# Four weight pieces' low parts formed by GpSimd instead of VectorE, beside the first batch's MLP

## What is computed

```python
def _moe2_ref(x, w_ch1, w_ch2) -> np.ndarray:
    X = np.fft.fft(x, axis=1)
    X = np.fft.fft(X, axis=2)
    mixed = np.real(X).astype(np.float32)
    u = x + mixed
    mu = np.mean(u, axis=-1, keepdims=True)
    var = np.mean((u - mu) ** 2, axis=-1, keepdims=True)
    un = (u - mu) / np.sqrt(var + 1e-06)
    ch = np.maximum(un @ w_ch1, 0.0) @ w_ch2
    return (u + ch).astype(np.float32)
```

## Time and profile before

| | us |
|---|---|
| median of 3 runs | 588.84 |
| lowest, highest | 588.84, 588.99 |
| the profiled execution, whole | 591.47 |
| its span, first to last instruction | 589.7 |

### The profile page before, as it was taken

One profiled execution on the slowest core, in us unless ns is written; L12 is line 12 of the kernel. 1 busy time (PEld: TensorE's weight loads), 2 busy tenths in 40 slices (PEclk: granted clock), 3 DMA queues, 4 the chain that ended last, 5 costly groups with the idle time before them and its releaser, 6 DMA issues.

```text
span 589.7 us, 12408 instructions
## 1 busy us (share of the span) xinstructions
PE 573.9 (97%) x5173; PEld 544.0 (92%) x5173; DVE 399.8 (68%) x891; ACT 199.1 (34%) x441; POOL 14.0 (2%) x31
## 2 busy tenths in 40 slices
PE   7999999999999999999999999999999999999996
PEld 6788999999999999999999999999999999999995
DVE  7579989978948676886948476877855574542221
ACT  4333355424333144324133133322433223322220
POOL 0000000000000000000000000000000000000000
PEclk7999999999999999999999999999999999999999
DMA  7658001232222002043202002022100000000000
GB/s 273 220 160 372 1 19 53 70 113 73 71 79 71 27 1 70 20 122 97 70 5 93 28 2 70 2 92 94 53 1 28 1 27 2 1 1 28 10 18 27
DMA packets 16858, 37.84 MB, mean 64 GB/s; under 512 B 2337, under 2 KB 5410, under 8 KB 16546
## 3 DMA queue, kind: packets, MB, share of 16 engines
q1 hardware_dynamic: 14976, 32.32, 16.2%
q0 software_dynamic: 1536, 4.72, 2.2%
q10 hardware_dynamic: 290, 0.01, 0.0%
HBM read 32.32 MB, written 4.72 MB: 63 GB/s over the span
## 4 chain that ended last, share of the span: by engine, by line
PE 91%; DVE 5%; issue 2%; ACT 1%; DMA 0%; POOL 0%; DVEq 0%
PE bank L897 44%; PE bank L982 24%; PE evens L929 4%; PE sums L938 3%; PE bank L1008 2%; PE evens L954 2%; PE evens L962 2%; PE evens L967 2%; PE bank L1079 2%; PE sums L924 1%; PE bank L1045 1%; PE bank L1089 1%; PE bank L1014 1%; DVE unT_lo L648 1%; PE evens L957 1%
## 5 line engine op out<-in xcount | busy, mean ns | idle before, releaser
L879 DVE SCALAR_TENSOR_TENSOR h_lo<-bank,h_hi 128x256 fp32r<-128x256 f32 x144 | 60.6, 422 | 100.7 <-ACT h_hi L641 98.0
L897 PE MATMUL bank<-unT_hi,w_hi 128*128 128x256 f32 x432 | 125.4, 290 | 2.7 <-DVE unT_lo L648 2.2
L897 PE MATMUL bank<-unT_lo,w_hi 128*128 128x256 f32 x432 | 122.1, 283 | 0.0
L897 PE MATMUL bank<-unT_hi,w_lo 128*128 128x256 f32 x432 | 121.6, 282 | 0.0
L641 ACT ACTIVATE h_hi<-bank 128x256 fp32r<-128x256 f32 x144 | 54.9, 381 | 174.0 <-PE bank L897 174.0
L982 PE MATMUL bank<-w_hi,h_hi 128*128 128x384 f32 x288 | 99.3, 345 | 0.0
L982 PE MATMUL bank<-w_lo,h_hi 128*128 128x384 f32 x288 | 97.6, 339 | 0.0
L982 PE MATMUL bank<-w_hi,h_lo 128*128 128x384 f32 x288 | 97.2, 338 | 0.0
L897 PEld LDWEIGHTS bank<-unT_hi,w_hi 128*128 128x128 f32 x432 | 81.2, 188 | 9.3 <-DVE unT_lo L648 4.9
L897 PEld LDWEIGHTS bank<-unT_hi,w_lo 128*128 128x128 f32 x432 | 81.6, 189 | 0.0
L897 PEld LDWEIGHTS bank<-unT_lo,w_hi 128*128 128x128 f32 x432 | 81.4, 189 | 0.0
(11 more groups left out here) (186 smaller groups left out, 1078.6 us busy)
## 6 DMA issues: line engine op xcount, KB each, us to landing
a_in<-in_alpha_dram SPq DMA_DIRECT2D x24, 258.5 KB, 2.7
q_in<-in_q_dram SPq DMA_DIRECT2D x24, 256.0 KB, 2.7
k_in<-in_k_dram SPq DMA_DIRECT2D x24, 256.0 KB, 3.1
v_in<-in_v_dram SPq DMA_DIRECT2D x24, 224.0 KB, 3.3
w_raw<-in_w_dram SPq DMA_DIRECT2D x2, 2304.0 KB, 11.6
out_dram<-u POOLq DMA_DIRECT2D x24, 192.0 KB, 2.3
dftd<-in_dft_d_dram SPq DMA_DIRECT2D x1, 582.0 KB, 6.4
woutT<-in_w_out_t_dram SPq DMA_DIRECT2D x1, 576.0 KB, 7.2
```

The source lines that it names most:

```text
L879: dve.scalar_tensor_tensor(h_lo[:, f % HBUF, :], ps[:, 0:GW], 0.0, h_hi[:, f % HBUF, :].bitcast(F32), ALU.max, ALU.subtract).then_inc(s_re ...
L897: last = pe.matmul(ps, l, r, start=(i == 0), stop=(i == len(mms) - 1))
```

## The change

A new kind of step, `wlp`, replaces `wlo` at the four places in the first batch's MLP, in the same slots of the list. VectorE doesn't know the kind and passes it over; GpSimd does the same subtraction on the same 128x1536 elements, after a wait for ScalarE's high part, and counts a semaphore of its own. PE waits for that semaphore ahead of `h` 4, `down` 4, `h` 8 and `down` 8 of the first group. The first pieces, and all other weights, stay with VectorE.

```diff
@@ mlp(b)
         for a, j, name in plan["wlo"]:
             slots[a - 1] += [("whi", 0, WN.index(name), j)]
-            slots[a] += [("wlo", 0, WN.index(name), j)]
+            slots[a] += [("wlp", 0, WN.index(name), j)]
@@ gpsimd
             for w in SCHEDULE:
                 kind, b, a, f = w
-                if kind == "out":
+                if kind == "wlp":
+                    pool.wait_ge(s_whi, WHI_AT["whi", 0, a, f] + 1)
+                    raw, high, low = (part(w_[WN[a]], a, f) for w_ in (w_raw, w_hi, w_lo))
+                    pool.tensor_tensor(low, raw, high.bitcast(F32), ALU.subtract).then_inc(s_wlp, 1)
+                elif kind == "out":
@@ tensor
             def weight_ready(name, j=0):
 
-                pe.wait_ge(s_wlo, WLO_AT["wlo", 0, WN.index(name), j] + 1)
+                if j > 0:
+                    pe.wait_ge(s_wlp, WLP_AT["wlp", 0, WN.index(name), j] + 1)
+                else:
+                    pe.wait_ge(s_wlo, WLO_AT["wlo", 0, WN.index(name), j] + 1)
```

More of the change, by code:

```diff
@@ L217 @@
     DREAD_AT["pqe", b_, 0, 0] = DREAD_AT["pqo", b_, 0, 0]
-WHI_AT, WLO_AT = order_of("whi"), order_of("wlo")
+WHI_AT, WLO_AT, WLP_AT = order_of("whi"), order_of("wlo"), order_of("wlp")
 def bank_plan():
@@ L409, in build @@
         s_wlo = sem("weights_lo")
+        s_wlp = sem("weights_lo_by_gpsimd")
         s_in = [sem("qk_loaded_even"), sem("qk_loaded_odd")]
```

## The result

| us | before | changed |
|---|---|---|
| median | 588.91 (4 runs) | 597.18 (4 runs) |
| lowest, highest | 588.84, 588.99 | 595.48, 598.74 |
| the profiled execution: whole, span | 591.47, 589.7 | 598.74, 597.0 |

The ratio is 1.014, with a 95% interval of 1.010 to 1.018: the change makes the kernel 8.3 us slower by the medians. The range on record, 588.6 to 594.6 us, missed it.

A forecast was written before the change was run, and what follows sets the result against it. PE was taken to bound the kernel, VectorE following close behind. Terms: 0 for what is taken away, + 2.2 + 0 + 0 + 0 for the four pieces, moving the median from 588.84 to 591.0 us; range 588.6 to 594.6.

The forecast's parts named there:

- What is taken away: Four VectorE subtractions in the first MLP, 7.0 us; no PE instruction waits for them, so worth 0 on the path.
- A piece takes 3.5 us on GpSimd: Each moved subtraction of 1536 elements per partition, priced at 12 times a 0.292 us GpSimd operation: 3.5 us.
- GpSimd and VectorE exclude each other for a whole instruction: GpSimd reading SBUF and VectorE instructions with two SBUF inputs: one waits completely for the other; chance 0.42.
- rival (a): GpSimd beside VectorE: no hindrance or only slight slowing, swallowed by the leads; 588.8 us, chance 0.27.
- Piece 1 of `w1`: GpSimd gets in ahead of L714, making it 3.5 us late; PE stalls 2.2 us at h 3.
- It must let L714 and L715 pass: Piece 2 (w2) gets in only after both, with h_lo 1 at 100.8 us; no further stall.
- rival (b): Turns at every instruction, piece 2 between L714 and L715: stall 5.7 us at h 3, 594.5 us, chance 0.22.
- the lead: Time from h_lo 1's end on VectorE to PE's start of h 3, which absorbs delay: 1.3 us.
- The difference carries over: Whole program: the profiled execution's 2.6 us above the median stays, so the median goes from 588.84 to 591.0 us.
- Pieces 3 and 4: Third pieces of w1 and w2, run after L776 and L777 and between L761 and L770: no stall, 0 each.
- the forecast's own order: GpSimd's piece 1 ahead of L714, piece 2 after L715, piece 3 after L776 and L777; 2.2 us in all.
- The other side: Faster: gaps between PE's groups might hide VectorE lateness, bringing back some tenths of a microsecond; 588.5 us or less, chance 0.04.

The follow-up runs named there:

- e7: Changed kernel with w1's third piece back on VectorE and the other three let go only behind chosen VectorE instructions: 590.52 us median, ratio 1.0011.
- e1: Changed kernel with only the second piece of w1 on GpSimd, the other three back on VectorE: 591.16 us median, ratio 1.0032.
- e2: Changed kernel with each of the four GpSimd pieces cut into six instructions of 256 elements: 590.18 us median, ratio 1.0014.
- e9: Changed kernel with GpSimd's second piece of w2 held back until after h_lo 1: 592.47 us median, ratio 1.0063.
- e11: The kernel of e9 run once more, unchanged, for a third profile: 592.18 us in one run.
- e4: Changed kernel with only the third pieces of w1 and w2 on GpSimd, the second ones back on VectorE: 597.5 us median, ratio 1.0133.
- e3: Changed kernel with 40 matmuls into an unused bank ahead of h 3, filling most of PE's gap: 594.31 us median.
- e10: The kernel of e9 run once more, unchanged, for a second profile: 592.34 us in one run.

## Why the prediction was wrong, point by point

**What is taken away is worth 0: right.** The kernel with three of the pieces at harmless places (e7) has 5.2 us less in VectorE's list and the levels of the kernel before, no better ones.

**A piece takes 3.5 us on GpSimd: right.** 3.51 us measured where nothing is in its way (e1). That 12 times the 0.292 us of the earlier trace rows came so close is luck: it scales up another operation with one input and its fixed part, and six parts of 256 elements at 0.72 us or more take 4.3 us or more (e2), not 3.5. The estimate from the Trainium skill (GPSIMD Engine Reference, section 3.1), 3.4 us, agrees as well, and is worked out from the same operation.

**GpSimd and VectorE exclude each other for a whole instruction: right.** Taken from the Trainium skill (SBUF — State Buffer, "Who interferes with whom"), and now shown: 3.73 against 0.56 us, 0.97 with sixths, nothing with fills. Rows with one input in PSUM go free as it says, e.g. `h_lo` at 0.42 during the third and fourth piece. The time without it, 588.8, was my rival (a) with 0.27; it is out.

**Piece 1 of `w1`, a stall of 2.2 us: right for one piece, some 0.3 too large.** 591.1 us in e1, a wait of 1.75 us there and of 1.76 to 1.80 in e9 to e11. GpSimd was 0.2 us ahead of L719, which the walk left out, and L719 lost 3.2 us instead of 3.5.

**"It must let L714 and L715 pass": this step failed.** I took it that VectorE, going from one such instruction to the next without a break, would keep GpSimd out, and read that from the overlap of their rows. That the rows overlap doesn't tell who may read next. GpSimd's second piece was waiting, and got in between: 3.77 us for L720 where 0.55 was assumed, so that the stall of 2.2 us became one of 5.15. This is rival (b), with 0.22 and 594.5 us; its 5.7 us, 7.0 less the lead, were measured as 6.4 less the lead. The runs that tell it: e1 (one piece, L720 at 0.55), e9 to e11 (the second piece held back, L722 at 0.55), e4 (the same double wait, 4.01 and 3.90, in front of other instructions).

**The half clock: not in the prediction at all, and this put the time outside the range.** I priced every stall at its own length. After the gap TensorE ran at 1.2 GHz for some microseconds, which cost 1.9 us in the first profile and 2.7 in the second one. The profile of before has a sign that PE can lose its clock when it has gaps: in its first 10 us PE was busy 6.5 us, and then comes this stretch (as above, PEclk is the third number from the end):

```profile
10.00:15.00 5.00, 5.00 (x51) 4.05 (x48) 3.88 (x8) 0.47 (x3) 0.00 (x0) 0.50 0.62 241
```

It is a sign and no rule, as the profiles at the quick start have the same work in their first 15 us at full clock. With this term rival (b) gives 588.8 + 5.2 + 1.9 to 2.7, some 596 to 597 us at the quick start, where 595.5 to 596.8 were measured; the two runs at 598.6 to 598.7 have the slower start on top. With the gap filled and the clock up (e3) it is 594.1 to 594.4, inside the range.

**"The difference carries over": wrong as a constant.** The 2.6 us between the profiled run (591.47) and the median (588.84) lie inside the span, 589.7 against about 587.1; both have 1.75 us outside it. They are the distance between the third level of the start and the first, and carry over only where both kernels are taken at the same levels. The median of the changed kernel, 597.18, is the middle of two runs at 595.6 and two at 598.7.

**Pieces 3 and 4, no stall: right in the changed kernel, wrong in the forecast's own order.** I let piece 3 wait until L776 and L777 were both through, the same step as above. e10 and e11 have my order and show the piece in between (4.00 us for L784), 1.0 us of wait for PE; so the walk should have given 2.2 + 1.2 (the second term as e10 measured it), 592.2 us, even with L714 and L715 passing together. In the changed kernel the long gap and the half clock had moved the piece behind both. Begun just ahead of them it costs all of it, in e4: 597.5 us.

**The other side**, faster, had 0.04, and no run showed anything of it.

## What to carry to other kernels

Work moved to GpSimd isn't free for VectorE if it reads SBUF. Look up which VectorE instructions with two SBUF inputs may meet it, take up to a whole GpSimd instruction of delay for each of them in a row, and compare the sum, not one of them, with the lead of what VectorE delivers next. And price a stall of PE with what the clock takes after it, here nothing to 1.6 us on top of a gap of 1.8 us, and 1.9 to 3.1 on gaps of 4.7 to 5.0 us. If such work has to be there, cut it in short instructions or let each begin behind one of VectorE's collisions; but where VectorE holds nobody up, as here, there is nothing to be won by relieving it: even the best placed version (e7) only equals the kernel before.

## What the runs showed of the hardware that I had not expected

- Turns: a waiting GpSimd instruction gets in between two VectorE instructions with two SBUF inputs each (3.73 and 3.77 us; 4.01 and 3.90 us; 0.68 and 4.00 us; with sixths 0.97 and 1.09 us).
- A GpSimd copy with one SBUF input delays VectorE's two-input instructions as well (1.06 and 1.18 us), a fill doesn't (0.56 and 0.55 us).
- VectorE's `TENSOR_SCALAR` on two elements with one SBUF input waited for GpSimd too, 2.39 us instead of 0.17, until the piece was through (105.03). The Trainium skill (SBUF — State Buffer, "Who interferes with whom") counts `tensor_scalar` among those that can take both ports; this row agrees.
- TensorE's clock fell to its half after a gap of 1.76 us in one execution of e9's kernel and stayed up in two others of the same kernel (1.77 and 1.80 us) and in e1 (1.75 us); after gaps of 4.7 to 5.0 us it fell in all three profiles, and with the gap filled by matmuls it stayed at 1.00. What decides it for the short gap is open.
